# Two score groups of a gated attention scan joined into one of 64 columns, with a new slot table and a new split of the weights' low parts

## What is computed

```
state = alpha[t] * state + outer(k[t], v[t])   # per batch and head, 768 steps
y[t]  = q[t] @ state
x = y with the heads side by side              # 3072 tokens x 384
x = (h - tanh(h)) @ w_out1,  h = x @ w_in1     # inner width 2048
x = (max(h,0) + a*min(h,0)) @ w_out2,  h = x @ w_in2
```

## Time and profile before

| | |
|---|---|
| profiled execution | 939.7 us, its span 937.3 us |
| three runs | 940.84, 939.42, 939.60 us |
| PE / PEld | 909.7 us (97% of the span) / 750.7 us |
| DVE / ACT / POOL | 565.3 / 310.6 / 210.2 us |
| chain that ended last | PE 96%, issue 1%, DVE 1%, ACT 1%, DMA 1% |
| granted PE clock | 1.0 in every stretch |

### The profile page before, as it was taken

How to read it: one execution, slowest core, us unless ns; L and a number is a source line. 1 busy time by engine, 2 the same in 40 slices (tenths; PEclk the granted TensorE clock), 3 DMA queues, 4 the chain that set the end, 5 groups by cost and what they waited for, 6 DMA issues and landing times.

```text
span 937.3 us, 24236 instructions
## 1 busy us (share of the span) xinstructions
PE 909.7 (97%) x10686; PEld 750.7 (80%) x10686; DVE 565.3 (60%) x706; ACT 310.6 (33%) x516; POOL 210.2 (22%) x196
## 2 busy tenths in 40 slices
PE   3799999999999999999999999999999999999998
PEld 3677888888888888888888888888888888888886
DVE  6779848664875676486434465555555655554553
ACT  5634532253234235322544531211211211212212
POOL 5683603331351334033304430000000000000000
PEclk9999999999999999999999999999999999999999
DMA  8370062026003500520054010020100100100000
GB/s 274 84 255 2 3 165 86 2 43 207 4 3 77 174 2 18 155 80 3 2 186 152 0 68 1 1 67 0 54 13 0 67 0 0 67 0 0 34 1 34
DMA packets 23529, 55.89 MB, mean 60 GB/s; under 512 B 3056, under 2 KB 11248, under 8 KB 20912
## 3 DMA queue, kind: packets, MB, share of 16 engines
q1 hardware_dynamic: 23296, 54.02, 18.7%
q10 hardware_dynamic: 144, 0.52, 0.2%
HBM read 40.90 MB, written 9.44 MB: 54 GB/s over the span
## 4 chain that ended last, share of the span: by engine, by line
PE 96%; issue 1%; DVE 1%; ACT 1%; DMA 1%; POOL 0%; SPq 0%; DVEq 0%; POOLq 0%
PE ph L651 43%; PE acc L660 14%; PE acc L662 14%; PE acc L661 14%; PE ps L484 4%; PE py L544 1%; PE ps L544 1%; PE py L540 1%; PE ps L540 1%; PE ps L472 1%; PE ps L479 1%; DMA q_early<-q 1%; PE acc L484 0%; DVE w_lo L1017 0%; PE py L607 0%
## 5 line engine op out<-in xcount | busy, mean ns | idle before, releaser
L831 ACT ACTIVATE g_hi<-g 128x512 fp32r<-128x512 f32 x192 | 121.2, 631 | 434.1 <-PE acc L662 336.6
L1042 DVE TENSOR_TENSOR g_lo<-g,g_hi 128x512 fp32r<-128x512 f32 x192 | 147.1, 766 | 188.0 <-ACT g_hi L831 187.2
L660 PE MATMUL acc<-g_lo,w_hi 128*128 128x512 f32 x576 | 227.3, 395 | 0.0
L662 PE MATMUL acc<-g_hi,w_hi 128*128 128x512 f32 x576 | 224.6, 390 | 0.0
L661 PE MATMUL acc<-g_hi,w_lo 128*128 128x512 f32 x576 | 224.6, 390 | 0.0
L651 PE MATMUL ph<-x_hi,w_lo 128*128 128x512 f32 x576 | 166.1, 397 | 0.0
L651 PE MATMUL ph<-x_lo,w_hi 128*128 128x512 f32 x576 | 162.2, 390 | 0.8 <-DVE x_lo L910 0.8
L651 PE MATMUL ph<-x_hi,w_hi 128*128 128x512 f32 x576 | 162.3, 390 | 0.0
L660 PEld LDWEIGHTS acc<-g_lo,w_hi 128*128 128x128 f32 x576 | 108.2, 188 | 24.5 <-DVE g_lo L1042 1.8
L651 PEld LDWEIGHTS ph<-x_lo,w_hi 128*128 128x128 f32 x576 | 108.1, 188 | 23.9 <-DVE x_lo L910 1.2
L651 PEld LDWEIGHTS ph<-x_hi,w_hi 128*128 128x128 f32 x576 | 108.2, 188 | 23.0
(11 more groups left out here) (128 smaller groups left out, 588.9 us busy)
## 6 DMA issues: line engine op xcount, KB each, us to landing
v_t<-v SPq DMA_DIRECT2D x6, 1024.0 KB, 6.8
a_t<-alpha SPq DMA_DIRECT2D x5, 1024.0 KB, 5.1
k_t<-k SPq DMA_DIRECT2D x5, 1024.0 KB, 6.9
x<-x_out SPq DMA_DIRECT2D x6, 768.0 KB, 8.7
x_in<-x SPq DMA_DIRECT2D x6, 768.0 KB, 5.1
kT<-trees SPq DMA_DIRECT2D x64, 64.0 KB, 2.0
q_w<-q SPq DMA_DIRECT2D x10, 384.0 KB, 5.5
out<-prob SPq DMA_DIRECT2D x5, 768.0 KB, 3.8
```

Source lines behind the costliest of these rows:

```text
L660: pe.matmul(acc[:, m, :], w_hi[:, f, part], g_lo[:, f % 2, :], start=(f == 0), stop=False)
L662: mm = pe.matmul(acc[:, m, :], w_hi[:, f, part], g_hi[:, f % 2, :], start=False, stop=(f == NF - 1))
L831: act.activation(g_hi[:, f % 2, :], g[:, f % 2, :], ACT.Copy).then_inc(g_hi_made, 1)
L1042: dve.tensor_tensor(g_lo[:, f % 2, :], g[:, f % 2, :], g_hi[:, f % 2, :].bitcast(F32), ALU.subtract).then_inc(g_lo_made, 1)
```

## The change

Groups 2 and 3 become one group, called 3, of 64 products of 64 columns (a whole block of 32 steps of two heads), so a tile has seven groups, `GROUPS`. For this the host lays q out in the order 1, 0, 2, 3 in every four steps. Group 1 reads places 1 and 2 of each four (steps 0 and 2), group 3 reads all four places: ACT first copies place 3 over place 1 (`swap`), DVE multiplies places 2 and 3 by their alphas (`begin`), and group 3 waits for that. Step 0 of each four is loaded once more into `q0_t`, multiplied there by DVE, and copied to place 1 after group 3. Group 3 fills both banks of ps, so it waits for mask 1, and group 4 for masks 2 and 3, which both read group 3's scores.

The low parts of weights are made by DVE for f = 0 to 2, by POOL for 3 to 6, and by DVE for 7 to 15 at the slots of `W_LO_BESIDE`. Weight slices 9 to 12 are loaded before tile 1's q and not after it. In tile 0 ACT and POOL share the clearing of q_w's pads, each lane's first products of q are halved and parted, and DVE makes x_lo in another order around w_lo 0 to 2.

```diff
-
-E_SLOTS = {1: (3, 6, 9, 13, 16, 19, 21, 24), 2: (3, 5, 8, 12, 15, 18, 20, 23), 3: (3, 6, 10, 13, 15, 18, 20, 23),
-           4: (3, 5, 9, 12, 15, 18, 20, 23), 5: (3, 7, 9, 11, 13, 16, 20, 23)}
+GROUPS = (1, 3, 4, 5, 6, 7, 8)
+
+
+E_SLOTS = {1: (3, 6, 10, 13, 16, 19, 22), 2: (3, 7, 11, 14, 17, 20, 23), 3: (3, 7, 11, 14, 17, 20, 23),
+           4: (3, 7, 11, 14, 17, 20, 23), 5: (3, 7, 11, 14, 17, 20, 23)}
...
+    for e, h in zip(GROUPS, E_SLOTS[a]):
+        if e > 1:
...
+        kinds = ["first"] if e == 1 else ["second", "grow"] if e == 3 else ["grow"]
+        for kind in kinds:
+            slots[h if late else h + 1].append((kind + "_late" if late else kind, e - 1))
+        if e == 1:
+            slots[h + 1].append(("mask", 1))
+        if e == 3:
+            slots[h + 1] += [("mask", 2), ("mask", 3)]
+        if 3 < e <= 6:
+            slots[h + 2].append(("mask", e))
...
-W_BEFORE = {2: [0], 3: [1, 2, 3], 4: [4, 5], LEVELS + 2: [6, 7]}
-
-
-W_EARLY = 9
+W_BEFORE = {2: [0], 3: [1, 2, 3], 4: [4, 5, 6], LEVELS + 2: [7, 8]}
+W_BESIDE = {0: [9], 1: [10], 7: [11], 10: [12], 17: [13], 22: [14], 23: [15]}
+
+
+W_EARLY = 13
 W_LO_FIRST = 3
-W_BESIDE = {0: [8], 3: [9], 5: [10], 7: [11], 8: [12], 9: [13], 11: [14], 13: [15]}
+W_LO_GPSIMD = 7
+W_LO_BESIDE = {0: [7], 1: [8], 2: [9, 10], 8: [11], 11: [12], 18: [13], 23: [14], 24: [15]}
...
             def load_tile(a):
...
+                past(sp, swapped[LANES], SWAPPED * n)
+                sp.dma_start(q0_t[:, :], q0[bass.ds(a * 128, 128), :]).then_inc(ld_q0, 16)
...
+                mm.then_inc(scored[set_of(lane)], 2 if e == 3 else 1)
+
+            def even(q):
+                return lambda x, t: q[:, x, :, t].rearrange("p s (n four) -> p s n four", four=4)[:, :, :, 1:3]
+
+            def whole_block():
+                return lambda x, t: q_w[:, x, :, t]
...
             def first_scores(lane, l):
...
-                    group(lane, 2, plain(q_early, 1))
-                    pe.wait_ge(pads_cleared, 2)
-                pe.wait_ge(q_grown[lane], 2 * l)
-                pe.wait_ge(masked[lane], l - 1)
+                    pe.wait_ge(pads_cleared[lane], 2)
+                    pe.wait_ge(swapped[lane], 2)
+                    pe.wait_ge(q_begun[lane], 2)
+                    group(lane, 3, whole_block())
+                    return
+                if l == 3:
+                    pe.wait_ge(q_begun[lane], LANE_Q_BEGUN)
+                pe.wait_ge(q_grown[lane], 2 * (l - 2))
+                pe.wait_ge(masked[lane], 1 if l == 3 else l - 1)
...
             def scores(a, e):
...
+                if e == 3:
                     pe.wait_ge(state_made, STATES * a)
                     pe.wait_ge(k_grown[LANES], K_GROWN * n + K_PARTS)
-                    group(None, 2, plain(q_w, 1))
+                    pe.wait_ge(q_begun[LANES], Q_BEGUN * n + 4)
+                    pe.wait_ge(swapped[LANES], SWAPPED * n + 2)
+                    pe.wait_ge(masked[LANES], MASKED * n + 1)
+                    group(None, 3, whole_block())
                     return
...
+                if e == 4:
+                    pe.wait_ge(q_begun[LANES], Q_BEGUN * (n + 1))
+                    pe.wait_ge(swapped[LANES], SWAPPED * (n + 1))
+                pe.wait_ge(q_grown[LANES], Q_GROWN * n + 2 * (e - 3))
+                pe.wait_ge(masked[LANES], MASKED * n + max(e - 2, 3))
...
+            def copy_plain(lane):
+
+                xs = xs_of(lane)
+                act.wait_ge(ld_q[lane], 32)
+                for hh in range(2):
+                    rows = slice(64 * hh, 64 * hh + 64)
+                    act.activation(fours(q_w[rows, xs, hh, :])[:, :, :, 0:2], fours(q_early[rows, xs, hh, :])[:, :, :, 0:4:3],
+                                   ACT.Copy).then_inc(swapped[lane], 1)
+
+            def swap(n, step):
+
+                act.wait_ge(scored[LANES], SCORED * n + (3 if step else 1))
+                if step:
+                    act.wait_ge(token0_made, n + 1)
+                for hh in range(2):
+                    rows = slice(64 * hh, 64 * hh + 64)
+                    to = fours(q_w[rows, :, hh, :])
+                    frm = q0_t[rows, :].rearrange("p (x n) -> p x n", x=X) if step else to[:, :, :, 3]
+                    act.activation(to[:, :, :, 1], frm, ACT.Copy).then_inc(swapped[LANES], 1)
...
-                    if what == "level" and l == 1 and lane == 1:
-                        copy_first_factors(lane)
+                    if what == "level" and l == 1 and lane == 0:
+                        copy_plain(lane)
...
+                    if what == "level" and l == 1 and lane == 0:
+                        copy_first_factors(1, False)
+                        copy_first_factors(1, True)
+                        copy_plain(1)
...
-            copy_first_factors(0)
-            act.wait_ge(zeroed, 2)
+            copy_first_factors(0, False)
+            act.wait_ge(zeroed, 4)
             clear_pads()
+            copy_first_factors(0, True)
...
+            def begin_lane(lane, step):
...
+                at = slice(0, 2) if step else slice(2, 4)
...
+                    by = first_factors(lane, step)[rows].rearrange("p (x n) two -> p x n two", x=XL)
+                    dve.tensor_tensor(fours(q_w[rows, xs, hh, :])[:, :, :, at], fours(q_early[rows, xs, hh, :])[:, :, :, at],
+                                      by, ALU.mult).then_inc(q_begun[lane], 1)
+
+            def start_lane(lane):
+
+                dve.wait_ge(ld_q[lane], 32)
+                dve.wait_ge(left_copied[lane], LANE_FACTORS)
+                begin_lane(lane, 0)
+
+            def begin(place, by, sem):
+
+                for hh in range(2):
+                    rows = slice(64 * hh, 64 * hh + 64)
+                    at = fours(q_w[rows, :, hh, :])[:, :, :, place]
+                    dve.tensor_tensor(at, at, by[rows].rearrange("p (x n) -> p x n", x=X), ALU.mult).then_inc(sem, 1)
...
+                if e <= 3:
+
+                    to = fours(near[:, heads, :])[:, :, :, (slice(1, 3), slice(0, 4, 3), slice(2, 4))[e - 1]]
+                    if e == 1:
+                        frm = scores_of(lane, 1).rearrange("p (h n two) -> p h n two", h=count, two=2)
+                    else:
+                        frm = scores_of(lane, 3).rearrange("p (h n four) -> p h n four", h=count, four=4)[
+                            :, :, :, 2 * e - 4:2 * e - 2]
+                    by = near_masks[:, e - 1, :] if e < 3 else near_masks[:, e - 1, :].bitcast(U32)
+                    by = by.rearrange("p (n two) -> p n two", two=2).unsqueeze(1).to_broadcast([128, count, NEAR // 4, 2])
+                    if e < 3:
+                        dve.tensor_tensor(to, frm, by, ALU.mult).then_inc(done, 1)
+                    else:
+                        dve.copy_predicated(to, by, frm).then_inc(done, 1)
...
             def first_tile(work):
...
+                        weights([0])
...
-                        weights([0])
                         x_low(0)
+                        x_low(1)
                         weights([1])
-                        x_low(1)
                     if what == "Y" and lane == 1:
-                        if l == 0:
+                        x_low(DUO + l)
+                        if l == 1:
                             weights(range(2, W_LO_FIRST))
-                        x_low(DUO + l)
...
+                    if l == 2:
+                        begin_lane(lane, 1)
+                        dve.wait_ge(q_begun[lane], LANE_Q_BEGUN)
+                    else:
+                        dve.wait_ge(q_grown[lane], 2 * (l - 2))
                     grow(lane, l, False)
                     if l == 2:
+                        if lane == 0:
+                            start_lane(1)
...
             def attention(work, a):
...
+                    if what in ("first", "first_late"):
+                        dve.wait_ge(ld_a[LANES], 16 * (n + 1))
+                        dve.wait_ge(scored[LANES], SCORED * n + 1)
+                        by_fours = a_t[:, :].rearrange("p (n four) -> p n four", four=4)
+                        begin(2, by_fours[:, :, 2], q_begun[LANES])
+                        dve.wait_ge(tree_made[LANES], TREE * n + 1)
+                        dve.wait_ge(swapped[LANES], SWAPPED * n + 2)
+                        begin(3, tree[1].rearrange("p (n two) -> p n two", two=2)[:, :, 1], q_begun[LANES])
+                        dve.wait_ge(ld_q0, 16 * (n + 1))
+                        dve.tensor_tensor(q0_t[:, :], q0_t[:, :], by_fours[:, :, 0], ALU.mult).then_inc(token0_made, 1)
+                    if what in ("second", "second_late"):
+                        dve.wait_ge(scored[LANES], SCORED * n + 3)
+                        begin(0, tree[1].rearrange("p (n two) -> p n two", two=2)[:, :, 0], q_begun[LANES])
...
-                weights([f for f in W_BESIDE.get(h, []) if f >= W_EARLY])
+                weights(W_LO_BESIDE.get(h, []))
```

153 lines of the change are left out of this document (76 added, 77 removed).

## The result

The changed kernel takes 967.3 us (966.1 to 968.2, six runs) against 939.6 for the kernel before in the same runs (938.4 to 940.8): a ratio of 1.029, 95% interval 1.028 to 1.031. Its profiled execution took 968.2 us, the span 966.4. The prediction was 946 (935 to 953): right in direction, off by 21 us and outside its range.

The account below looks back on a forecast made before the run. PE bounds the kernel, busy 85.96 of 86.00 us beside tile 2, so its own work and waits count. 939.7 + 1.6 (to tile 1's end) + 5.2 (tiles 2 to 5) = 946.5, given as 946, range 935 to 953.

Parts of the forecast that it names:

- Step 1: Joining groups 2 and 3 on PE: two of 1.46 us become one of 2.26, -0.66 us a tile (-0.40 to -1.46).
- Step 2: Tile 0: fewer PE records and stops, first product of pass 0 2.1 us earlier, at 43.6 us; bounds 0 and -4.
- what I costed at nothing: ACT's four copies a tile, the load of q0_t, and the earlier loads of slices 9 to 12: no time.
- Step 3: Into tile 1: DVE stands behind POOL, PE waits 6.1 us through group 3; +1.6 us to tile 1's end.
- Step 4: Group 3 in tiles 2 to 5: q products held by POOL make mask 1 late, PE waits 0.75 us each.
- rival C: DVE's q products stepping over four elements take double time, delaying masks 1 and 3: 970 us; chance 6%.
- Step 5: Group 4 in tiles 2 to 5: PE waits 1.2 us each for masks 2 and 3; bounds 0 and 1.9.

Follow-up runs that it names:

- the run with both parts left out: The spread version with q products and q0_t's product on contiguous elements and no load of q0_t after tile 1; 941.8 us (1.0019).
- with contiguous places: The changed kernel with the q products and q0_t's product on contiguous elements of spare tensors, q_w left unmultiplied there; 953.5 us (1.0129).
- the run with a short POOL: The changed kernel with POOL's two level 1 instructions growing k in tiles 1 to 5 cut to a thirty-second of the elements; 955.4 us (1.0175).
- the spread version: The changed kernel with groups 3 and 4 later, DVE's work spread over slots 3 to 12, before's low-part split and q_early start; 949.9 us (1.0097).

## Why the prediction was right or wrong, step by step

**Step 1 (joining): right.** The joined group takes 2.01 us at full clock. What it costs is best read in tile 2 of the run with both parts left out (941.8 us), from one `in` slot to the next:

```profile
157.95 0.84 PE L699 MATMUL ph<-x_hi,w_lo 128*128 128x512 f32 x3
...
164.04 0.96 PE L699 MATMUL ph<-x_hi,w_lo 128*128 128x512 f32 x3
...
168.25 0.84 PE L699 MATMUL ph<-x_hi,w_lo 128*128 128x512 f32 x3
```

Two slot pairs take 6.09 + 4.21 us, and 2 x 4.08 without a group, so the group costs 2.14 where two of 1.46 were: -0.78 for -0.66. In tile 2 of the changed kernel the same working gives 2.24, and -0.68. The Trainium skill (TensorE: Matmul & The Clock Gate, section Back-to-back issue gap) gives 1 to 64 columns equal time. It does not hold for these products, 2.14 us against 1.46, and the 7.3 us that it promised for five tiles were not there.

**Step 2 (tile 0): wrong.** The first product of pass 0 came at 46.28, not 43.6. PE's stops in the middle of a group are indeed fewer, three of 3.9 us together for five of 8.5, but what I costed at nothing took their place: slices 9 to 12 lengthen the stops (0.8 to 1.7 us in two runs), and between group 3 and group 4 of a lane DVE now has q products ahead of the growing:

```profile
14.78 1.40 DVE L943 TENSOR_TENSOR q_w<-q_early,acc 64x512 f32<-64x512 f32 x2 [1.70 <-PE ps L511]
16.22 1.40 DVE L967 TENSOR_TENSOR q_w<-q_w,py 64x512 f32<-64x512 f32 x2
```

That is 1.40 us more ahead of group 4, and PE waits 2.30 us for it. ACT's high parts run almost without a gap up to the placing at 32.21. The split alone in the kernel before, which brings the loads and the added high part with it, made tile 0 3.2 us longer, 1.5 more than the loads alone. How much each of these holds in the changed kernel is not settled, nor why a_t is first used 1.1 us later, at 7.12.

**Step 3 (tile 1): the mechanism right, the size short.** g_lo 0 ended at 58.76, 12.5 us behind the first product (predicted 12.4), because DVE stood behind POOL, idle for 5.65 us. The waits are 7.84 us for 6.1; with contiguous places the one ahead of group 3 is 3.17 for 5.05, so the places make 1.9 of it. At the end of tile 1 the change stood at +9.1 and not +1.6: 2.7 us of that are tile 0 and 1.7 waiting; the other 3 are left to the clock, which was at its lower level for part of this stretch (0.55 from 59.1 to 62.6 us and 0.52 from 72.8 to 79.7, in 7.9 us of busy PE).

**Step 4 (group 3): the term that failed.** 0.75 us were 2.8, by 0.76 + 0.76 + 0.42 us of slow places (4.26 for 3.50, 2.20 for 1.44 and 1.07 for 0.65) that the earlier trace rows did not show, since there q steps over two elements. That is rival C at half its price, given 6%. I had both ends (no cost, twice) and took the one end: the sum counted nothing for a form of operand that no row showed, though the pairs of before already read every second element. At half its price C gives 946.5 + 0.5 x 23.5 = 958, still 9 us short. By the run with contiguous places this term, with the clock and the stops that its waits brought, is about 14 us of the time. (A small slip: 155.55 - 154.85 is 0.70, not 0.75.) The turns with POOL are as forecast: 2.06 us before, 2.04 by the run with a short POOL (4.26 to 2.22). The Trainium skill (SBUF — State Buffer, section Who interferes with whom) has this as an exclusive lock of the shared port, and the trace agrees with these 2.04 us.

**Step 5 (group 4): the mechanism right where it could show, the size short.** 2.07 us in tile 2 for 1.2, beyond its bound of 1.9; with contiguous places it was 1.43. In tiles 3 to 5 PE came to group 4 later than forecast and found the mask done: in tile 3 it needed 12.24 us from the start of group 3, where tile 2 took 10.40, as the slower clock and, in tiles 4 and 5, the stops make it. So the 4.8 us became 2.07.

**What no step had: the clock and the stops.** Of the 28.5 us up to tile 5's end, 19.8 are waits for DVE, 4.2 stops, -3.4 the joinings, -2.2 waits and stops of before that went, and 0.6 tile 0. The rest is 9.5, and it is PE at a lower granted clock. In tile 3, for one, behind the wait of 2.78 us:

```profile
256.30:259.30 3.00, 3.00 (x129) 2.66 (x128) 1.92 (x4) 1.56 (x4) 0.00 (x0) 0.69 0.02 8
259.30:268.40 9.10, 9.10 (x36) 7.15 (x36) 8.28 (x8) 4.00 (x5) 4.75 (x3) 0.92 0.01 3
268.40:277.00 8.60, 8.57 (x270) 7.17 (x271) 6.96 (x9) 2.95 (x6) 3.09 (x3) 1.00 0.01 2
```

0.31 x 3.0 + 0.08 x 9.1 = 1.7 us, and that tile is 1.8 longer than its wait and its joining make it. These are means over the two levels, 1.2 and 2.4 GHz; a narrower window has the lower one:

```profile
258.00:260.00 2.00, 2.00 (x47) 1.73 (x40) 1.41 (x2) 1.50 (x3) 0.67 (x1) 0.50 0.01 4
```

There are five such places, with granted clocks of 0.57 to 0.59: 59 to 63, 72 to 80, 257 to 261, 345 to 353 and 441 to 445 us. PE is busy 23.1 us in them, which makes some 9.9 us lost, near the 9.5 that were left. Each begins in or within 1.5 us behind a wait or stop of PE of about 2 us or more; tile 2, with waits of 2.81 and 2.07, has none. A price of a wait by its length alone, as in my whole sum, is too low by about a half in this kernel.

Of what I costed at nothing, ACT's copies took 1.17 us each in tile 2 and not 0.6, but ended before DVE or PE came to them. The load of q0_t was not nothing: 3.2 us in the spread version.

**No version here beats the kernel before** by what can be told; x_lo's order alone is level with it. The best that computes all with the joined group is the spread version with the loads in before's order, 948.6 us; even without the slow places and q0_t's loads, and with before's split, it is 941.8. The joining is worth 3.4 to 3.9 us in five tiles and needs three more DVE instructions and four more of ACT a tile, a transfer, and a later table.

## What to carry to other kernels

Before a DVE operand is made to step over more elements, measure one such instruction: the price here was half again, on the engine that decides the next group. Where PE is 97% busy, price a wait at its length plus the clock behind it, and ask of a burst on another engine not only who waits for its end but what stands behind it in that queue. And before reading a difference of some per cent as the change's doing, shift PE's instruction stream by a few dozen products: a position alone was worth 20 us of 940.

## What the hardware showed that I had not expected

- Products of 64 x 512 elements on DVE: 0.70 us contiguous and 0.72 in steps of two, 1.10 in steps of four; 128 x 512 with one of three operands in steps of four 1.07 for 0.69.
- PE's stops about every 127 matmul records: 0.4 to 3.5 us each where they are not hidden, in both kernels. 32 more products ahead of them hit other products with them and cost 20 us; transfers of 256 KB a tile that nobody waits for brought three of them.
- In or behind most waits of PE of 2.5 to 5 us the granted clock fell to its lower level, 0.50, for some microseconds, also behind a stop of 3.54 us of the kind "issue"; behind the waits of tile 2 (2.81 and 2.07 us) it did not. In tiles 2 to 5 of the spread version of 949.9 us, with waits of at most 0.73 us and stops of at most 1.39, it stayed at 1.00.
- In tile 0 the clock counted for little: two traces with the same start of PE's stream, one at 1.00 and one at 0.50 from 20 to 43 us (q0_t's load left out), had their first product of pass 0 at 46.66 and 46.48 us.
